# A two-mixture kernel on one core: the low product of the last 64 rows of layer 1 as pairs of 64-row matmuls

## What is computed

```python
def _moe_ref(x, w_gate, w1, w2):            # the second mixture takes two experts per row, with noisy gates
    logits = x @ w_gate
    expert_idx = np.argmax(logits, axis=1)
    ...
    for e in range(E):
        xe = x[expert_idx == e]
        h = np.maximum(xe @ w1[e], 0.0)
        ye = h @ w2[e]
        out[mask] = gate_w[mask, None] * ye

def reference(**kwargs):
    attn_out = _attn_ref(**attn_kwargs)     # softmax over 7 taps per head, causal, depthwise
    x = attn_out.reshape(B * S, D)
    x = _moe_ref(x=x, **moe_kwargs)
    return _moe2_ref(x=x, **moe2_kwargs)
```

## Time and profile before

| | |
|---|---|
| median of 3 runs | 2038.46 us (2037.15 to 2040.99) |
| the profiled execution | 2038.28 us, of it 2036.5 us from first to last instruction |
| TensorE matmul busy | 1908.1 us (94%) |
| VectorE busy | 1216.6 us (60%) |
| ScalarE busy | 847.5 us (42%) |
| GpSimd busy | 942.5 us (46%) |
| mean granted TensorE clock | 0.978 |

### The profile page before, as it was taken

One profiled execution on the slowest core, in us unless ns is written; L12 is line 12 of the kernel. 1 busy time (PEld: TensorE's weight loads), 2 busy tenths in 40 slices (PEclk: granted clock), 3 DMA queues, 4 the chain that ended last, 5 costly groups with the idle time before them and its releaser, 6 DMA issues.

```text
span 2036.5 us, 49899 instructions
## 1 busy us (share of the span) xinstructions
PE 1908.1 (94%) x14519; PEld 1853.4 (91%) x14520; DVE 1216.6 (60%) x4101; ACT 847.5 (42%) x2019; POOL 942.5 (46%) x1174
## 2 busy tenths in 40 slices
PE   7990899999999999789999999999999999999998
PEld 4760899999999999789999999999999999999998
DVE  6551677777777777745555554545555554555554
ACT  2430454444454444433443443433433433434333
POOL 4777244444444444434444444444444444444444
PEclk9995899999999999989999999999999999999999
DMA  6642332332332323222222232221322222312221
GB/s 224 205 158 76 102 113 86 113 113 82 112 102 91 111 86 106 72 92 62 64 89 61 66 91 65 85 74 60 99 61 62 93 62 65 98 60 78 79 63 48
DMA packets 113044, 184.90 MB, mean 91 GB/s; under 512 B 21516, under 2 KB 89092, under 8 KB 110848
## 3 DMA queue, kind: packets, MB, share of 16 engines
q1 hardware_dynamic: 72576, 104.32, 16.8%
q0 software_dynamic: 40320, 79.90, 12.0%
q10 hardware_dynamic: 128, 0.46, 0.1%
HBM read 111.73 MB, written 76.97 MB: 93 GB/s over the span
## 4 chain that ended last, share of the span: by engine, by line
PE 52%; DMA 2%; issue 1%; DVE 1%; POOL 0%; POOLq 0%; DVEq 0%; ACT 0%; ACTq 0%; SPq 0%
PE bank L998 17%; PE bank L999 8%; PE bank L983 5%; PE bank L979 5%; PE bank L980 5%; PE bank L981 5%; PE bank L982 5%; DMA so_far<-out,at_n 1%; PE bank L966 1%; PE bank L968 1%; DMA out<-y,at_c 1%; DVE y L720 0%; DVE y L713 0%; DVE h_l L724 0%; POOL out L1150 0%
## 5 line engine op out<-in xcount | busy, mean ns | idle before, releaser
L998 PE MATMUL bank<-w2hl,h_h 128*128 128x384 f32 (+1 forms) x2832 | 859.6, 368 | 20.3 <-DVE h_l L724 20.3
L999 PE MATMUL bank<-w2hl,h_l 128*128 128x192 f32 (+1 forms) x2832 | 720.3, 254 | 0.0
L998 PEld LDWEIGHTS bank<-w2hl,h_h 128*128 128x128 f32 x2832 | 532.3, 188 | 25.8 <-DVE h_l L724 24.8
L724 DVE SCALAR_TENSOR_TENSOR h_l<-bank,h_h 128x512 fp32r<-128x512 f32 x708 | 468.1, 688 | 138.5 <-ACT h_h L472 119.4
L999 PEld LDWEIGHTS bank<-w2hl,h_l 128*128 128x128 f32 x2832 | 541.6, 191 | 0.0
L472 ACT ACTIVATE h_h<-bank 128x512 fp32r<-128x512 f32 x708 | 421.6, 596 | 277.3 <-PE bank L983 277.2
L979 PE MATMUL bank<-x_h,w1mh 128*128 128x256 f32 x1416 | 402.8, 284 | 3.4 <-DVE x_h L684 3.4
L983 PE MATMUL bank<-x_h,w1ll 128*128 128x256 f32 x1416 | 402.1, 284 | 0.0
L980 PE MATMUL bank<-x_l,w1mh 128*128 128x256 f32 x1416 | 399.5, 282 | 0.0
L982 PE MATMUL bank<-x_h,w1lh 128*128 128x256 f32 x1416 | 399.2, 282 | 0.0
L981 PE MATMUL bank<-x_h,w1ml 128*128 128x256 f32 x1416 | 399.0, 282 | 0.0
(11 more groups left out here) (185 smaller groups left out, 1927.8 us busy)
## 6 DMA issues: line engine op xcount, KB each, us to landing
rows<-rows_of_mixture SPq DMA_DIRECT2D x179, 208.0 KB, 2.6
raw<-in_w_of_both SPq DMA_DIRECT2D x17, 1024.0 KB, 6.3
raw<-in_w_of_both SPq DMA_DIRECT2D x17, 768.0 KB
x_in<-in_x SPq DMA_DIRECT2D x16, 768.0 KB, 4.7
out<-zeros SPq DMA_DIRECT2D x61, 192.0 KB
rows_of_mixture<-row,pos POOLq DMA_INDIRECT x244
rows_of_mixture<-pad_rows SPq DMA_DIRECT2D x18, 208.0 KB, 2.1
so_far<-out,at_n POOLq DMA_INDIRECT x232, 2.8
```

What stands on the lines that cost most here:

```text
L724: V.scalar_tensor_tensor(h_l[:, 2 * p:2 * p + 2, :].rearrange("p c t -> p (c t)"), bank[1 + p][:], 0.0, h_h[:, 2 * p:2 * p + 2, :].rearran ...
L998: T.matmul(dst, h_h[:, c, tok], both, start=(c == 0), stop=False)
L999: last = T.matmul(bank[5 + a][:, 0:width], h_l[:, c, tok], w2hl[:, c, 0:width], start=False, stop=(c == F // P - 1))
```

## The change

x_s is a new tile: on partitions 0 to 63 a copy of the high part (ScalarE), on 64 to 127 the low part (VectorE). It takes the place of the stacked half of x_h in the product with w1lh. x_h's second half now keeps the high part on both halves of the partitions. The product with w1ll is made of two matmuls over 64 rows, one on partitions 0 to 63 for the block of one bank, one on 64 to 127 for the block of the next bank; low by low is no longer computed. Layer 1 goes over the first halves of all banks and then over the second halves, and in mixture 1 the routing steps stand in other places between the ReLUs.

```diff
                 def split_x(s):
                     act.wait_ge(xt2_done[m], s + 1)
                     nc.scalar.activation(x_h[:], bank[0][:], ACT.Copy).then_inc(xh_ready[m], 1)
+                    act.wait_ge(xh_ready[m], s + 1)
+                    nc.scalar.activation(x_s[0:DL, :], x_h[0:DL, SLOT:2 * SLOT], ACT.Copy).then_inc(xs_ready[m], 1)
...
                 def body(s, e, last):
+                    if m == 0:
+                        softplus(s)
+                        keep_y(s)
                     for p in range(PAIRS):
                         relu(s, p)
                         if last:
                             split_w1_h(E * m + e + 1, p)
-                        if p == 0 and m == 0:
-                            softplus(s)
                         if p == 1:
                             left_twice(s + 1)
-                        if p == 2 and m == 0:
-                            keep_y(s)
                     split_x(s + 1)
...
-                    V.tensor_tensor(x_h[DL:P, SLOT:2 * SLOT], bank[0][DL:P, SLOT:2 * SLOT], x_h[DL:P, SLOT:2 * SLOT],
+                    V.tensor_tensor(x_s[DL:P, :], bank[0][DL:P, SLOT:2 * SLOT], x_h[DL:P, SLOT:2 * SLOT],
                                     ALU.subtract).then_inc(xl_ready[m], 1)
...
-                    between = (add_noise, find_two, mark_two) if m == 0 else ()
+                    if m == 0:
+                        add_noise(s, link)
+                        find_two(s, link)
                     for p in range(PAIRS):
                         relu_l(s, p)
                         if last:
                             split_w1_l(E * m + e + 1, p)
-                        if p < len(between):
-                            between[p](s, link)
+                        if p == 1 and m == 0:
+                            mark_two(s, link)
...
+                def layer1(s, e):
+
+                    pe.wait_ge(xl_ready[m], s + 1)
+                    pe.wait_ge(xs_ready[m], s + 1)
+                    main, low = x_h[:, 0:SLOT], x_h[:, SLOT:2 * SLOT]
                     for i in range(2):
+                        lanes = [(bank[1 + p][:, i * SLOT:(i + 1) * SLOT], slice((2 * p + i) * P, (2 * p + i + 1) * P)) for p in range(PAIRS)]
+                        for p, (dst, f) in enumerate(lanes):
+                            if i == 0:
+                                pe.wait_ge(w1_ready, PAIRS * (E * m + e) + p + 1)
+                            T.matmul(dst, w1mh[:, f], main, start=True, stop=False)
+                            T.matmul(dst, w1mh[:, f], x_l[:], start=False, stop=False)
+                            T.matmul(dst, w1ml[:, f], main, start=False, stop=False)
+                            T.matmul(dst, w1lh[:, f], x_s[:], start=False, stop=False)
+                            if p % 2:
+                                for half, (dst, f) in ((slice(0, DL), lanes[p - 1]), (slice(DL, P), lanes[p])):
+                                    last = T.matmul(dst, w1ll[half, f], low[half, :], start=False, stop=True)
+                                    if i:
+                                        last.then_inc(l1_done[m], 1)
```

More of the change, by code:

```diff
@@ L160, in attention_and_two_mixtures @@
         x_l = sb("x_l", [P, SLOT], f32r)
+        x_s = sb("x_s", [P, SLOT], f32r)
         h_h, h_l = sb("h_h", [P, F // P, SLOT], f32r), sb("h_l", [P, F // P, SLOT], f32r)
@@ L209, in attention_and_two_mixtures @@
         w1_ready, w2_ready = sem("w1_ready"), sem("w2_ready")
-        rows_loaded, rows_ready, xt2_done, xh_ready, xl_ready = two("rows_loaded"), two("rows_ready"), two("xt2_done"), two("xh_ready"), two("xl_ready")
+        rows_loaded, rows_ready, xt2_done, xh_ready, xl_ready, xs_ready = two("rows_loaded"), two("rows_ready"), two("xt2_done"), two("xh_ready"), two("xl_ready"), two("xs_ready")
         l1_done, hh_ready, hl_ready, l2_done = two("l1_done"), two("hh_ready"), two("hl_ready"), two("l2_done")
@@ L969, in transpose_rows @@
                     last.then_inc(xt2_done[m], 1)
-                def layer1(s, e, p):
-                    if p == 0:
-                        pe.wait_ge(xl_ready[m], s + 1)
-                    pe.wait_ge(w1_ready, PAIRS * (E * m + e) + p + 1)
+                def layer1(s, e):
+                    pe.wait_ge(xl_ready[m], s + 1)
+                    pe.wait_ge(xs_ready[m], s + 1)
+                    main, low = x_h[:, 0:SLOT], x_h[:, SLOT:2 * SLOT]
                     for i in range(2):
-                        dst = bank[1 + p][:, i * SLOT:(i + 1) * SLOT]
-                        f = slice((2 * p + i) * P, (2 * p + i + 1) * P)
-                        main, stacked = x_h[:, 0:SLOT], x_h[:, SLOT:2 * SLOT]
-                        T.matmul(dst, w1mh[:, f], main, start=True, stop=False)
-                        T.matmul(dst, w1mh[:, f], x_l[:], start=False, stop=False)
-                        T.matmul(dst, w1ml[:, f], main, start=False, stop=False)
-                        T.matmul(dst, w1lh[:, f], stacked, start=False, stop=False)
-                        last = T.matmul(dst, w1ll[:, f], stacked, start=False, stop=True)
-                    last.then_inc(l1_done[m], 1)
+                        lanes = [(bank[1 + p][:, i * SLOT:(i + 1) * SLOT], slice((2 * p + i) * P, (2 * p + i + 1) * P)) for p in range(PAIRS)]
[11 more added lines that the diff above has]
+                                        last.then_inc(l1_done[m], 1)
                 width = WY if m == 0 else D
@@ L1015, in body @@
                 def body(s, e):
-                    for p in range(PAIRS):
-                        layer1(s, e, p)
+                    layer1(s, e)
                     transpose_rows(s + 1)
```

## The result

The changed kernel takes **2225.39 us** (median of 4 runs, 2224.33 to 2225.81), the kernel before, beside it on the same chip, 2037.81 us. The ratio is 1.0917, 95% interval 1.0898 to 1.0936. The forecast was 2176 in a range of 2105 to 2235: the sign and the kind of cost were right, the size 49 us short, and the result lies outside the range that the favoured case had for itself (2130 to 2200). One execution of the kernel before, beside e5 to e8, took 8618.62 us and is left out.

A forecast was written before the change was run, and what follows sets the result against it. The prediction took TensorE's own matmul stream to bound plain slots. Pairs +136, left half's copy +20 and routing -18 summed to +138 on 2038, giving 2176 us, range 2105 to 2235.

The forecast's parts named there:

- the favoured case: Whole kernel: 64-row pairs pay borders and their halves overlap; 2176 us, own range 2130 to 2200, chance 0.66.
- the case without overlap: Rival for the 64-row pairs: second matmul a whole step behind, borders paid; 2219 us, chance 0.16.
- Border in, 0.09 + 0.02: Layer 1, entering each 64-row pair: 0.09 us late start plus 0.02 us for the open weight load.
- Second matmul 0.06 later: Within a pair: second matmul starts 0.06 us behind the first; a 4 ns start would make the sum about 42 us smaller.
- the low bound: Within a pair: second matmul starts at once, 0 us behind the first; then +0.13 us per pair and +94 us.
- What the loads cost at a border, 0.02 and 0.05: Layer 1, around each pair: weight loads lying open add 0.02 us going in and 0.05 us coming out.
- Sum per pair +0.19: Layer 1, each of 708 pairs: 0.43 us against 0.238 before, +0.19 us, together +136 us.
- Left half's copy, nil in plain slots and +20: Transposes waiting for the copy after layer 1: about nil in plain slots, 1.3 us in 16 last slots, +20 us.
- Routing, -18: Moved routing steps: mask wait mostly gone, 13 us, and -5 us from h_l waits in mixture 2; -18 us.
- x_s's copy hidden: The added 64x256 copy on ScalarE, once per slot: covered by the 16 pairs of layer 2, no cost.
- no border: Rival: 64-row tiles pay no border, but plain slots wait 0.41 us on the left half's copy; 2034 us, chance 0.07.
- full gain: Rival: no border, and the wait on the left half's copy hidden by unseen slack; 1941 us, chance 0.03.

The follow-up runs named there:

- e5: The change, with old layer 1 and full-row w1ll in each expert's first and last slot, one 64-row run elsewhere, left copy early; 2040.35 us, ratio 1.0016 to before.
- e8: The change with all eight 64-row matmuls of a slot in one run and the left half's copy ahead of the ReLUs; 2050.12 us, ratio 1.0064 to before.
- e2: The change with both 64-row matmuls of a pair on partitions 0 to 63; 2445.01 us on another chip, ratio 1.1484 to the kernel before.
- e11: The change with only the left half's copy moved ahead of the ReLUs; 2221.62 us, ratio 1.0901 to the kernel before.
- e10: The change with only the routing steps back in their old places; 2243.87 us, ratio 1.1004 to the kernel before.
- e1: The change with the w1ll product over all 128 rows again, its bank order and routing kept; 2326.22 us on another chip, ratio 1.0953 to before.
- e12: The change with full-row w1ll and the left half's copy ahead of the ReLUs, same kernel as e3 on another chip; 2069.97 us, ratio 1.0147 to before.
- e3: The change with full-row w1ll and the left half's copy ahead of the ReLUs; 2281.12 us on the chip of 2131.02 us, ratio 1.0711 to before.

## Why the prediction was right, and where it was short

The sign was right for the reason given: a border costs more than the step that a pair saves. The size is luck in part. The favoured case, borders with overlap, had 2130 to 2200 for itself, and the result is 25 us over that. It lies in the stated range because the upper end, 2235, was set for the case without overlap, which e2 refutes.

- **Border in, 0.09 + 0.02.** The first matmul of a pair starts 0.21 behind the last full one: the 0.09 read from the chunks of the first phase carries over to 64 rows (0.21 - 0.119 = 0.09). The 0.02 beside it was for the open load, which is the third point.
- **Second matmul 0.06 later.** It is at once, 3 ns. I had taken the value of the nearest row; the low bound was the right one. Overlap itself is shown by e2. (By the 4 ns of the sentence beside it the sum would be 0.056 x 708 = 40 us smaller, not 42.)
- **What the loads cost at a border, 0.02 and 0.05.** This is the step that failed. The gap behind the first matmul of the narrow run is 0.10 over a step (e8), and the gap behind the first full matmul again 0.10 (0.22 in place of 0.12). I had read it from L881 and L854, whose groups of four ended 0.02 and 0.05 late, and taken that as what is always left open. The gaps stand at the same two places there, behind the first matmul on each side, but with tiles of 32x32 and 112x112; why they are 0.10 with 128 columns of weights and 256 of data no run separates. A visit costs 0.38 to 0.40, where my terms give 0.09 + 0.02 + 0.09 + 0.05 = 0.25.
- **Sum per pair +0.19.** Measured: +1.05 / 4 = 0.26. 708 pairs at 0.07 more are 50 us, which is the miss (2225 - 2176 = 49): the open loads 0.13 more, the second matmul 0.06 less. The two errors offset each other in part, 92 us against 42; with the second matmul priced rightly I should have written 2134. For the same reason plain slots are at 11.21 and 10.84 us where I had 10.9 and 10.55.
- **Left half's copy, nil in plain slots and +20.** Right: 18.0 us in 16 places, and 0.09 us of room in plain slots. e11 adds that this wait cannot be bought off by moving the copy.
- **Routing, -18.** The sum is right, -19.1, its parts are not: the mask gives 9.1 us where I had 13, and h_l 10.0 where I had 5. The h_l part is not the routing's at all. It lies in mixture 2, which has no routing (11.2 us before, none after), because TensorE arrives later there; in mixture 1 it went up from 9.1 to 10.3. That e10 costs 18.5 us is a coincidence of size, since most of it is the left half's copy in plain slots.
- **x_s's copy hidden.** The change's wait on x_s is 3.4 us in all, as the wait of the same product on x_h was before, so it is.
- **Rivals.** No overlap is refuted by e2 and the 3 ns, no border and full gain by the 0.21, 0.32 and 0.22 of every pair. What I said would show the border free, a wait of about 0.4 on the copy in plain slots, came up as 0.24 in e1, which has no border.

That the 0.10 on each side is the weight load lying open, and the 0.09 TensorE emptying itself, is my reading: no run moved one without the other. For it stand the weight loads in the page after, with the one of L991's counterpart before in the last line (PEld; the last columns are the idle time ahead of them and what was waited for):

```profile
L985 PEld LDWEIGHTS bank<-x_h,w1mh 128*128 128x128 f32 x1416 | 267.2, 189 | 73.3 <-issue 5.0
...
L987 PEld LDWEIGHTS bank<-x_h,w1ml 128*128 128x128 f32 x1416 | 269.0, 190 | 0.0
...
L991 PEld LDWEIGHTS bank<-x_h,w1ll 64*128 64x128 f32 x1416 | 132.2, 183 | 96.8 <-issue 1.1
...
L983 PEld LDWEIGHTS bank<-x_h,w1ll 128*128 128x128 f32 x1416 | 268.5, 190 | 0.0
```

L991's and L985's lose their lead, with next to nothing named that they waited for; L987's keep it. The Trainium skill (TensorEngine Tiling (Array Packing), Key Properties) says that a change of tiling mode drains the engine; the 0.09 agree with that, and it gives no price.

## What to carry to other kernels

Price a change of tile shape per visit, not per matmul: here 0.40 us for going into 64-row tiles and back, against 0.119 saved by each pair, so a visit must hold at least four pairs, and one pair at a time loses. Grouping them moves the moment at which banks are ready, so keep the old order in the few slots where the consumers are already late. When a wait disappears by moving one step of a busy engine, look at what that engine delivers next: in e11 most of the wait came back there. And price a long wait with what follows it: in e5 the clock fell behind six of seven waits of 2.7 us and more, which cost 10 us, as much as the waits themselves had grown by.

## What the runs showed of the hardware that I had not expected

- Within a run of 64-row pairs the steps are 0.12 us, the same as full matmuls; only the second pair of the run is 0.10 late. So it is not the narrow matmuls themselves that are slow, but the place behind the border.
- Two 64-row matmuls on the same half (e2) are about 0.22 apart, not 0.12 (together 0.50, of which the second lasts 0.28): the same late second, on its own.
- After waits of TensorE of 1.7 to 3.0 us for h_l the granted clock fell to 1.2 GHz in some slots and not in others with the same wait (e5, e12); most falls cost 1.4 to 1.7 us each, read from slots with and without one.
- The kernel before took 2036.76 to 2037.86 us (medians) beside three of the four sets of runs and 2131.02 beside one, while plain slots of mixture 2 came out equal to the hundredth of a microsecond. In mixture 1 the granted clock there was 0.92 in the mean (e3), against 0.99 in the same kernel elsewhere (e12). What drew out mixture 1 stays open; ratios are taken within one chip only.
